# Raw weights of an ELU network's first layer loaded one piece per pair of chunks, into memory of the set-up, with the split parts stored the other way round

## What is computed

```python
# 1: delta-rule attention, batch 4, 8 heads, 768 steps, head size 48
k_n = k / (norm(k) + 1e-6)
for t in range(768):
    y[t]  = q[t] @ state
    state = state + beta[t] * outer(k_n[t], v[t] - k_n[t] @ state)
x = y as [3072 tokens, 384]
# 2: ELU network, w_in [384, 2048], w_out [2048, 384]
h = x @ w_in
x = where(h > 0, h, exp(min(h, 0)) - 1) @ w_out
# 3: top-2 of 8 experts with noisy gates, w1 [384, 1024], w2 [1024, 384] each
logits = x @ w_gate + log1p(exp(x @ w_noise)) * noise
out[token] += weight * (relu(x[token] @ w1[e]) @ w2[e])   # the two best e of each token
```

## Time and profile before

| | |
|---|---|
| median of 3 runs | 1171.54 us (1167.91, 1171.54, 1172.96) |
| the profiled execution's own time | 1170.35 us |
| its span in the trace | 1168.6 us |
| TensorE: matmuls, weight loads | 1116.6 us (96% of the span), 1069.0 us (91%) |
| VectorE, ACT, POOL | 647.9 (55%), 462.5 (40%), 355.3 (30%) us |
| chain that ended last | TensorE 74%, VectorE 1%, nothing else of 1% |
| DMA | 137.30 MB, 117 GB/s over the span; fullest slice of a fortieth (29 us) 370 GB/s |
| DMA queues | SP's 87.97 MB, POOL's 28.75 MB, ACT's 18.97 MB, "instruction" 1.36 MB in 83 packets and 0.25 MB in 30 |
| granted TensorE clock | 0.997 of full speed |

### The profile page before, as it was taken

One profiled execution on the slowest core, in us unless ns is written; L12 is line 12 of the kernel. 1 busy time (PEld: TensorE's weight loads), 2 busy tenths in 40 slices (PEclk: granted clock), 3 DMA queues, 4 the chain that ended last, 5 costly groups with the idle time before them and its releaser, 6 DMA issues.

```text
span 1168.6 us, 29044 instructions
## 1 busy us (share of the span) xinstructions
PE 1116.6 (96%) x11562; PEld 1069.0 (91%) x11562; DVE 647.9 (55%) x1552; ACT 462.5 (40%) x1048; POOL 355.3 (30%) x378
## 2 busy tenths in 40 slices
PE   4898999899999999999999999999999999999996
PEld 3886787778999999999999999999999999999995
DVE  4989788663455646465565647533534343434342
ACT  1236665784333333433333345423333333333331
POOL 4289995542002021020202012322222232322223
PEclk9999999999999999999999999999999999999998
DMA  7553556855997011110101011472424242424221
GB/s 158 127 126 93 132 120 155 220 159 199 370 358 241 21 48 41 35 41 20 41 20 41 15 50 65 172 231 76 165 74 173 76 168 84 157 97 145 62 70 53
DMA packets 82603, 137.30 MB, mean 117 GB/s; under 512 B 11050, under 2 KB 70034, under 8 KB 81466
## 3 DMA queue, kind: packets, MB, share of 16 engines
q1 hardware_dynamic: 68490, 87.97, 25.9%
q0 software_dynamic: 12992, 28.75, 7.6%
q10 hardware_dynamic: 1008, 18.97, 4.3%
HBM read 81.96 MB, written 53.77 MB: 116 GB/s over the span
## 4 chain that ended last, share of the span: by engine, by line
PE 74%; DVE 1%; issue 0%; ACT 0%; POOL 0%; ACTq 0%; POOLq 0%
PE ps_x L1409 18%; PE ps_x L1499 18%; PE ps_h L1398 17%; PE ps_h L1477 17%; PE ps_r L1457 2%; PE ps_r L1448 2%; DVE hg L1817 0%; ACT hg L1607 0%; POOL out_dram L1364 0%; DVE w_parts L1780 0%; PE ps_r L1516 0%; DVE x_raw L1810 0%; PE ps_r L1426 0%; ACT yT_d L1625 0%; PE ps_r L1424 0%
## 5 line engine op out<-in xcount | busy, mean ns | idle before, releaser
L1499 PE MATMUL ps_x<-hg,w_parts 128*128 128x400 f32 x1152 | 230.2, 346 | 0.0
L1409 PE MATMUL ps_x<-w_parts,hg 128*128 128x400 f32 x1152 | 229.7, 346 | 0.0
L1398 PE MATMUL ps_h<-xg,w_parts 128*128 128x384 f32 x1152 | 222.3, 338 | 0.0
L1477 PE MATMUL ps_h<-xg,w_parts 128*128 128x400 f32 x1116 | 220.6, 345 | 1.1 <-DVE w_parts L1780 1.1
L1409 PEld LDWEIGHTS ps_x<-w_parts,hg 128*128 128x128 f32 x1152 | 209.6, 188 | 0.0
L1817 DVE SCALAR_TENSOR_TENSOR hg<-ps_h,hg 128x400 fp32r<-128x400 f32 x128 | 73.6, 575 | 243.1 <-ACT hg L1607 242.6
L1398 PEld LDWEIGHTS ps_h<-xg,w_parts 128*128 128x128 f32 x1152 | 204.0, 188 | 2.5 <-DVE elu_parts L1674 2.5
L1477 PEld LDWEIGHTS ps_h<-xg,w_parts 128*128 128x128 f32 x1116 | 202.7, 188 | 4.0 <-issue 3.1
L1499 PEld LDWEIGHTS ps_x<-hg,w_parts 128*128 128x128 f32 x1152 | 206.0, 188 | 0.0
L1344 POOL DMA_INDIRECT xs_scratch<-x,rows_now x48 | 49.2, 1025 | 393.5 <-DVE rows_now L1754 293.9
L1607 ACT ACTIVATE hg<-ps_h 128x400 fp32r<-128x400 f32 x128 | 64.6, 505 | 256.4 <-PE ps_h L1477 256.4
(11 more groups left out here) (175 smaller groups left out, 1312.4 us busy)
## 6 DMA issues: line engine op xcount, KB each, us to landing
xs_scratch<-pads SPq DMA_DIRECT2D x2, 5502.0 KB, 42.4
x_rows<-xs_scratch SPq DMA_DIRECT2D x17, 614.1 KB
kqT<-in_kqT_dram SPq DMA_DIRECT2D x48, 192.0 KB, 4.0
carried<-in_w_dram ACTq DMA_DIRECT2D x3, 3072.0 KB, 10.9
w_raw<-in_w_dram ACTq DMA_DIRECT2D x3, 3072.0 KB, 11.3
xs_scratch<-pads SPq DMA_DIRECT2D x6, 1375.5 KB, 17.0
out_dram<-pads SPq DMA_DIRECT2D x1, 4800.0 KB, 30.3
xs_scratch<-pads SPq DMA_DIRECT2D x6, 786.0 KB, 8.9
```

Of the source, the lines that this page charges most:

```text
L1398: mm = nc.tensor.matmul(ps_h[f % 2][:, 0:TB], wi[:, a, k, f * P:(f + 1) * P], xr[:, b, k, :], start=(i == 0), stop=(i == len(passes) - 1))
L1409: mm = nc.tensor.matmul(ps_x[t][:, 0:DG], act_r[:, f % RING, a, t * P:(t + 1) * P], wo[:, b, f, :], start=(f == 0 and i == 0), stop=(f == ...
L1477: mm = nc.tensor.matmul(ps_h[f % 2][:, 0:TR], w1, xg[:, b, k, :], start=(m == 0), stop=(m == len(passes) - 1))
L1499: mm = nc.tensor.matmul(ps_y[k][:, 0:TR], w2r[i][:, a, s, k * P:(k + 1) * P], hg[:, s % RING, b, :], start=(s == 0 and m == 0), stop=(s == ...
```

## The change

Where SP issues each piece, by pair (a semicolon parts what follows the even chunk's reloads from what follows the odd's):

| pair | 1 | 2 | 3 | 4 | 5 | 6 | 7 | 8 | 9 | 10 |
|---|---|---|---|---|---|---|---|---|---|---|
| before | | | | | | | 0; 1, 2 | 3; 4, 5 | 6; 7, 8 | 9; 10, 11 |
| after | 2 | 3 | 4 | 5 | 0 | 1 | | 6 | 7; 8 | 9; 10, 11 |

The raw numbers of pieces 0 to 5 now go to the first half, columns 0 to 6144, over beta, gains, `kT` and the beginning of `gram`. SP waits for all lanes to be turned ahead of each, and for pieces 0 and 1 also for group 2 to be scaled and its norms turned. ACT writes their `hi` to the second half, and it is ACT that waits, before its first piece, for the last inverse and the placed chunks. POOL writes `lo` over the raw numbers in the first half. For pieces 6 to 11 everything lies as before. The network's first product takes `hi` and `lo` of `w_in` from the swapped halves. When ACT and POOL do their twelve pieces is not changed.

```diff
+W_EARLY = 6
+W_LOADED_WITH = {1: (2,), 2: (3,), 3: (4,), 4: (5,), 5: (0,), 6: (1,), 8: (6,), 9: (7, 8), 10: (9, 10, 11)}
...
-    w_raw = inversion[:, W_COLS:2 * W_COLS]
+    w_raw = inversion[:].rearrange("p (a c) -> p a c", a=2)
...
+        kT_at = cut_at
         kT = cut(KT_BUFS, 2 * NG, QP, P)
         gram = cut(NU, BLK)
+        assert W_CUTS[W_EARLY] <= cut_at
...
+        def raw_half(i):
+            return 0 if i < W_EARLY else 1
+        def piece_of(w, a, i):
+            return w[:, a, W_CUTS[i]:W_CUTS[i + 1]]
...
             def load_weights(i):
-                at, to = W_CUTS[i], w_raw[:, W_CUTS[i]:W_CUTS[i + 1]]
+                at, to = W_CUTS[i], piece_of(w_raw, raw_half(i), i)
...
-                if i == 0:
-                    for p in range(2):
-                        sp.wait_ge(inv_placed[p], W_PAIR * NR)
-                if i == W_EACH:
+                if i < W_EARLY:
+                    sp.wait_ge(to_lanes, NSET)
+                if W_CUTS[i] < kT_at:
+                    sp.wait_ge(scaled[GROUPS - 1], GSETS + 1)
+                    sp.wait_ge(norms_turned, GROUPS)
+                if i == W_EARLY:
                     sp.wait_ge(from_lanes, NSET)
                 sp.dma_start(to, given).then_inc(w_loaded[i], 16)
...
-                pieces = [(m - W_PAIR + 1) * W_EACH + i for i in range(W_EACH)] if W_PAIR - 1 <= m < PAIRS - 1 else []
+                pieces = W_LOADED_WITH.get(m, ())
...
-                        piece = slice(W_CUTS[i], W_CUTS[i + 1])
+                        a = raw_half(i)
                         pool.wait_ge(w_hi, i + 1)
-                        nc.gpsimd.tensor_tensor(wio[:, 1, piece], w_raw[:, piece], wio[:, 0, piece], ALU.subtract
+                        nc.gpsimd.tensor_tensor(piece_of(wio, a, i), piece_of(w_raw, a, i), piece_of(wio, 1 - a, i), ALU.subtract
                                                 ).then_inc(w_split, 1)
...
             def round_weights(i):
                 act.wait_ge(w_loaded[i], 16)
-                piece = slice(W_CUTS[i], W_CUTS[i + 1])
-                if piece.start == WI_COLS:
+                if i == 0:
+                    act.wait_ge(from_lanes, NSET)
+                    for p in range(2):
+                        act.wait_ge(inv_placed[p], W_PAIR * NR)
+                if i == W_EARLY:
                     act.wait_ge(gate_set, 1)
-                nc.scalar.activation(wio[:, 0, piece], w_raw[:, piece], ACT.Copy).then_inc(w_hi, 1)
+                a = raw_half(i)
+                nc.scalar.activation(piece_of(wio, 1 - a, i), piece_of(w_raw, a, i), ACT.Copy).then_inc(w_hi, 1)
...
-                    mm = nc.tensor.matmul(ps_h[f % 2][:, 0:TB], wi[:, a, k, f * P:(f + 1) * P], xr[:, b, k, :],
+                    mm = nc.tensor.matmul(ps_h[f % 2][:, 0:TB], wi[:, 1 - a, k, f * P:(f + 1) * P], xr[:, b, k, :],
```

More of the change, by code:

```diff
@@ L745, in set_gate @@
                 act.wait_ge(gate_taken, 1)
-                raw = w_raw[:, WI_COLS:W_COLS].rearrange("p (f d) -> p f d", d=DG)
+                raw = w_raw[:, 1, WI_COLS:W_COLS].rearrange("p (f d) -> p f d", d=DG)
                 nc.scalar.activation(raw[:, :, D:DG], gate.rearrange("p (f e) -> p f e", e=GATES), ACT.Copy
```

## The result

Six runs each, on one chip: 1171.24 us before (1167.91 to 1172.96), 1165.28 us after (1163.59 to 1167.03). The ratio is 0.9949 with a 95% interval of 0.9933 to 0.9966: 6.0 us or 0.51% faster. A repetition on another chip, one of the experiments, gave 0.9954 (0.9936 to 0.9972). The forecast was 1168.8, so the direction was right, the range just held the value, and the gain was a little more than twice the 2.7 us that I had worked out.

What follows compares the result with a forecast made beforehand. TensorE was taken to nearly bound each attention pair, with instruction breaks in pairs 8 and 9. Terms -3.3 + 0.6 + 0 = -2.7 us gave 1167.7 profiled, 1168.8 median; 8-in-10 range 1164.8 to 1173.8.

Steps and rivals of the forecast that it cites:

- The bound and the place: TensorE nearly bounds every pair of the attention stage; its unexplained idle time, 4.8 us, lies in pairs 8 and 9.
- the 2.7 that I had left of 3.3: Pairs 8 and 9: 3.3 us gained from breaks removed, less 0.6 for single loads that stay.
- the swap and the moved waits: Swapped halves and waits moved from SP to ACT: costed at nothing, 0.5 us for the range.
- The trace shows the order in time, not the cause.: Caution on reading pairs 8 and 9 as TensorE lacking instructions because their transfer stands behind data.
- rival A: Breaks in pairs 8 and 9 are not the weight loads' doing; 1171.5 us, chance 0.26 together with case D.
- The rule that I had put beside it: DMA engines alternate between queue rows packet by packet, so instruction transfers should not stand behind SP's backlog; would favour rival A.
- The wait that was to come back: Pairs 8 and 9: without breaks TensorE meets VectorE waits of 1.2 us a pair; gain 3.3 instead of 4.8.
- rival C: All breaks go, behind single loads too, and VectorE's waits do not return: -5.8 us or more, 1165.5; chance 0.08.
- ACT's rounding: ACT's 0.99 us wait for a load at its second piece goes: worth nothing, at most 1.0 us.
- Early loads at nothing: One 512 KB load in each of pairs 1 to 6: taken as 0, at most 7.6 us lost.
- Rival B: Slower through the same breaks in pairs 1 to 6; one in each gives +4.5 us, 1176.0; chance 0.12.

Runs made afterwards that it cites:

- e1: Changed kernel with all twelve loads back in their old places, leaving only the swapped halves and moved waits: 1171.38 us, ratio 0.9994 to the kernel before.
- e10: Changed kernel plus the six first-layer pieces loaded again at their old places into free columns, ACT waiting for the copies only ahead of piece 6: 1170.13 us, 0.9987.
- e7: Changed kernel with pieces 3, 4, 5 back in pair 8, 6 back in pair 9, and 2, 0, 1 in pairs 1, 5, 6: 1169.00 us, 0.9977.
- e8: As e1, with the six first-layer loads described as four 1 KB rows per partition instead of one of 4 KB: 1171.54 us, 0.9995.
- e3: Changed kernel with each of its six early loads issued twice, once into free columns, ACT waiting for both: 1169.83 us, ratio 0.9991 to the kernel before.
- e4: Changed kernel with pieces 0 and 1 moved from pairs 5 and 6 to the end of pair 7, issued together: 1169.99 us, 0.9987.
- e5: Changed kernel run again without any edit, on a second chip: 1167.33 us, ratio 0.9954 to the kernel before.
- e2: Changed kernel with its six early loads issued in twos behind the odd chunk's reloads of pairs 2, 4 and 6: 1167.33 us, 0.9958.
- e11: Changed kernel with pieces 6, 7, 8 issued one each in pairs 7, 8, 9 instead of 8, 9, 9: 1165.20 us, 0.9938.
- e6: Changed kernel with piece 1 alone moved from pair 6 to the end of pair 7: 1167.45 us, 0.9955.

## Why the prediction was right, and where it was not

*The bound and the place: right.* The chain, the windows by pair and TensorE's idle "issue" time pointed to pairs 8 and 9, and there 3.7 us went, against the 2.7 that I had left of 3.3. e1 finds nothing else in the change that counts, as I had costed the swap and the moved waits (its interval leaves room for up to 1.9 us); e10 that traffic of the weight loads makes the breaks.

*"The trace shows the order in time, not the cause."* It was the right caution and the right guess; rival A, with 0.26, is refuted as to the time by e1, e7 and e10. In one thing it was right: the places of the breaks are the program's own, and some breaks come with single loads too. The rule that I had put beside it is weighed differently now: the Trainium skill, "DMA: Bandwidth & Descriptors", on queues, rings and completion order, has each DMA engine go round its queue rows packet by packet, from which I drew that the loads' place would not matter. It does, by 4.1 us. Whether a transfer of instructions waits behind packets or behind bytes no run here tells, since e8's rows were joined. And the Trainium skill's "Runtime: NRT & Kernel Launch", instruction fetch mechanics, calls the fetch mostly hidden: in these traces it fails often behind bunched loads in pairs 7 and 8 (4.8 us in two pairs before and in e1, 5.1 in e10) and less often behind single ones (0.3 to 3.0 us in the same two pairs; 1.18 us in pair 2 of the changed kernel). It is no rule: e3's twos in pairs 1 to 3 had no break behind them ahead of pair 4.

*The wait that was to come back: wrong.* I cut 4.8 to 3.3 because TensorE would meet a VectorE wait of 1.2 us a pair where the breaks had covered it. In pairs 8 and 9 of the changed kernel these waits come to 0.3 us. That is rival C's reason ("VectorE's waits do not return"), to which I gave 0.08, and the median, 1165.28, is at its figure of 1165.5 and not at my 1168.8; only its first half fails, since 1.6 us of breaks stayed. By e10 the loads' traffic is worth 4.1 us where the sum had 2.7. That the range held the value owes something to luck: it lies 0.5 us from the edge.

*The other step that failed* is the one on ACT's rounding: "ACT is busy for only 12.7 of that pair's 18.1 us: nothing, at most 1.0". I read one profile's 0.99 us as the size of the thing, and ACT's share of busy time as slack. It is a wait for a transfer, whose length changes with when SP comes to the load and with which piece it is: 1.0, 1.2, 2.6 and 3.6 us in four traces with bunched loads (before, e1, e4, e8). In ACT's order the copy of the next solved block stands behind it and TensorE stands behind that; its waits for ACT in pair 8 of these traces are 0, 0.4, 1.1 and 2.7 us, the last with the clock at 1.2 GHz behind it. So for the execution that I had before me "nothing" was right, and as a mean it was not: e10 leaves 1.5 us for it, though with an interval that reaches down to 0.

*The rest of the difference* is in how the traced executions stand to the others. They show the network starting 3.5 us sooner, and 2.2 us in e5 (276.52 us), where the medians show 6.0 and 5.1. The changed kernel's two traced executions were 1.75 and 0.8 us above their medians, the old kernel's 0.9 below its own. The six executions of each scatter by 3.4 to 5.1 us. What the untraced ones look like is not known; e5, e8 and e10 show what can make 2 us or more, and some of the scatter is there before the pairs begin to differ: POOL's scaling in pair 1 comes at 103.39 in e1 and at 105.55 in e8, the same kernel.

*Early loads at nothing: right on the time, wrong on the reason.* I took 0 because the single load at 198.98 had no break behind it. In fact there was a break in pair 2, and twos in e2 brought 2.7 us of them. They cost little because POOL's chain of columns bounds these pairs up to its scaling in pair 6, and TensorE's lost time is taken from its waits in pairs 5 and 6. The cover has an end: in e10 the breaks of pair 6 cost 3.1 us. I had POOL's busy share (15.1 of 16.1 us) and read it only as a danger: it was the cover of everything early, and in e3, where the cover itself moved, the danger came true.

*Rival B* (slower through early breaks) did not happen, because the early breaks were few (none to three in the six traces that have the changed kernel's early loads) and mostly covered by POOL. e10's pair 6 shows that its danger was real: 3.1 us from single early loads at the changed kernel's own places, in one execution.

## What to carry to other kernels

When an engine is idle and the profile names no releaser, look at what the DMA queues carry just then, at the packets named "instruction" among it, and count the instructions between such places: a constant number says that it is the supply of instructions. Spreading bulk loads over a longer stretch can then help; here it was worth 0.5%. A wait seen once in one profile is a sample, not a bound, and if the waiting engine has in-order work behind it that others need, its low busy share is no cover. Before pricing a disturbance, find which engine's chain bounds that stretch; on the others it is free up to their slack.

## What the runs showed of the hardware

- TensorE can run out of instructions in straight-line code. It happened only at places some 251 instructions apart (matmuls and weight loads together), with a packet of the "instruction" queue served 2.4 to 3.5 us before TensorE went on.
- In pairs 8 and 9 the breaks came to 4.8, 4.8 and 5.1 us with bunched 512 KB loads in pairs 7 and 8 (before, e1, e10; 0.3 in e8, where TensorE had waited 2.7 us for ACT), to 1.8 and 2.4 with only one load of two in these pairs (e4, e7), and to 0.3 to 3.0 us with single ones. Single breaks were as long as 1.89 us behind bunched loads (e1) and 1.70 behind single ones (e10, pair 6).
- Of ten idle times of TensorE of 1.70 us and more in the pairs, six were followed by a granted clock at the lower level, 1.2 GHz, for some 3 to 6 us (1.70 in pair 6 of e10, 1.94 in e7, 2.15 in e5, 2.28 in e11, 2.74 in e8, 2.83 in e3), and four were not (1.75 in pair 8 of e10, 1.89 in e1, 2.13 in e2, 2.14 in pair 5 of e8). Two waits of 1.04 and 1.13 us in pair 1 of e6 were followed by it as well. The 48 matmuls of a solve took 1.53 us in such a stretch (e5) where they take 1.07. So a long wait often has a second price.
- Rows of 1 KB in a description of contiguous memory are joined again somewhere on the way: the packet count didn't change (e8).
- 3 MB more of loads, spread two to a pair over six pairs, delayed one 192 KB load of v by more than 2.4 us (e3; inferred).
